# Selection passes of VectorE in another order, and weight splits ahead of GpSimd's squares, in a fused attention and expert kernel

## What is computed

```python
scores = scale * np.matmul(q, k.transpose(0, 1, 3, 2))
kth = np.partition(scores, -32, axis=-1)[..., -32:-31]
scores = np.where(scores >= kth, scores, -1e9)
attn = softmax(scores)                      # max taken off, sum + 1e-9
x = rows_of(np.matmul(attn, v))             # (2304, 512)
h = np.maximum(x @ w_in, 0.0)
x = (h * h) @ w_out                         # 512 -> 2048 -> 512
skip = x @ w_skip > 0                       # rows that go to an expert
out[skip] = x + gate * (np.maximum(x @ w1[e], 0.0) @ w2[e])
```

## Time and profile before

| | |
|---|---|
| median of 3 runs | 930.87 us (929.56 to 931.46) |
| profiled execution | 931.42 us, its span 929.7 us |
| TensorE busy | 884.4 us (95%) |
| VectorE busy | 835.4 us (90%) |
| ScalarE busy | 659.5 us (71%) |
| GpSimd busy | 656.9 us (71%) |

### The profile page before, as it was taken

How to read it: one execution, slowest core, us unless ns; L and a number is a source line. 1 busy time by engine, 2 the same in 40 slices (tenths; PEclk the granted TensorE clock), 3 DMA queues, 4 the chain that set the end, 5 groups by cost and what they waited for, 6 DMA issues and landing times.

```text
span 929.7 us, 21066 instructions
## 1 busy us (share of the span) xinstructions
PE 884.4 (95%) x6674; PEld 718.1 (77%) x6674; DVE 835.4 (90%) x2584; ACT 659.5 (71%) x1297; POOL 656.9 (71%) x884
## 2 busy tenths in 40 slices
PE   3788799999999999999999999999999999999997
PEld 1677677788788877888878887887888887688886
DVE  6999999999999999999999999999993064888887
ACT  2777777787777777778777777877876322788886
POOL 1889888777787877878788787787878443344432
PEclk9999999999999999999999999999999999999999
DMA  8962544356544567966554445633533685764990
GB/s 309 370 226 80 180 152 123 122 180 190 182 141 145 162 230 240 248 206 197 178 172 142 149 149 175 211 123 105 194 115 114 227 274 188 268 244 143 346 339 10
DMA packets 69751, 175.40 MB, mean 189 GB/s; under 512 B 21299, under 2 KB 26419, under 8 KB 65281
## 3 DMA queue, kind: packets, MB, share of 16 engines
q1 hardware_dynamic: 67792, 168.91, 54.1%
q0 software_dynamic: 1840, 5.06, 1.7%
HBM read 154.19 MB, written 21.27 MB: 189 GB/s over the span
## 4 chain that ended last, share of the span: by engine, by line
PE 59%; DVE 35%; issue 3%; POOL 1%; ACT 1%; DMA 0%; SPq 0%; POOLq 0%; DVEq 0%
DVE top L1036 11%; DVE upper L1041 10%; PE psum L1330 5%; PE psum L1395 5%; PE psum L1396 5%; PE psum L1397 5%; DVE top L1051 5%; PE psum L1412 5%; PE psum L1413 4%; PE psum L1414 4%; PE psum L1355 4%; PE psum L1374 4%; DVE lower L1056 3%; DVE lower L1027 3%; PE psum L1627 2%
## 5 line engine op out<-in xcount | busy, mean ns | idle before, releaser
L1036 DVE MAX8 top<-upper 128x8 f32<-128x288 f32 x576 | 233.3, 446 | 0.0
L620 POOL TENSOR_TENSOR s_sb<-s_sb,below 128x576 f32<-128x576 f32 x144 | 203.5, 1436 | 2.0 <-ACT below L792 2.0
L1041 DVE MATCH_REPLACE8 upper<-top,upper 128x288 f32<-128x288 f32 x432 | 187.8, 442 | 0.0
L1395 PE MATMUL psum<-x_high,w_in_high 128*128 128x256 f32 x576 | 168.4, 292 | 1.6 <-POOL x_low L626 1.1
L783 ACT ACTIVATE s_sb<-psum 128x576 f32<-128x576 f32 x144 | 93.8, 651 | 103.9 <-PE psum L1330 92.5
L1396 PE MATMUL psum<-x_low,w_in_high 128*128 128x256 f32 x576 | 161.8, 281 | 0.0
L1397 PE MATMUL psum<-x_high,w_in_low 128*128 128x256 f32 x576 | 161.2, 280 | 0.0
L635 POOL TENSOR_TENSOR square<-relu 128x256 f32<-128x256 f32 x144 | 89.8, 624 | 80.9 <-ACT relu L825 80.7
L1330 PE MATMUL psum<-k_sb,q_sb 64*128 64x288 f32 x512 | 101.3, 472 | 32.9 <-DVE lower L1027 24.0
L640 POOL TENSOR_TENSOR g_low<-square,g_high 128x256 fp32r<-128x256 f32 x144 | 108.6, 754 | 29.4 <-POOL square L635 20.4
L792 ACT ACTIVATE below<-s_sb,steep_kth 128x576 f32<-128x576 f32 x144 | 110.9, 770 | 8.3 <-POOL neg_max L608 6.7
(11 more groups left out here) (213 smaller groups left out, 1876.6 us busy)
## 6 DMA issues: line engine op xcount, KB each, us to landing
w_ring<-w_split SPq DMA_DIRECT2D x144, 512.0 KB, 4.6
weights<-w SPq DMA_DIRECT2D x32, 1024.0 KB, 6.0
v_sb<-v_main SPq DMA_DIRECT2D x48, 256.0 KB, 2.6
w_split<-w_ring SPq DMA_DIRECT2D x16, 512.0 KB, 3.1
k_sb<-kT SPq DMA_DIRECT2D x32, 144.0 KB, 4.6
k_sb<-kT SPq DMA_DIRECT2D x32, 128.0 KB, 4.4
q_sb<-qT SPq DMA_DIRECT2D x32, 128.0 KB, 4.2
weights<-w_out SPq DMA_DIRECT2D x1, 4096.0 KB, 13.4
```

The costliest lines, as they stand in the source:

```text
L620: nc.gpsimd.tensor_tensor(s_sb[:, s % SBUFS, n, 0:S], s_sb[:, s % SBUFS, n, 0:S], below[:, n, :], ALU.subtract).then_inc(masked, 1)
L1036: v.max(top[:, s % 2, n, 8 * r:8 * r + 8], upper[:, s % 2, n, :]).then_inc(upper_step, 1)
L1041: v.match_replace(upper[:, s % 2, n, :], top[:, s % 2, n, 8 * r:8 * r + 8], upper[:, s % 2, n, :], LOWEST).then_inc(upper_step, 1)
L1395: t_.matmul(dst, wh, x_high[:, j % 2, k, :], start=k == 0, stop=False)
```

## The change

Two orders change; no instruction is added or taken away.

On VectorE the last passes of step t and the first two of step t+1 are interleaved. Before, the end of a step read `upper_max(t,3,0)`, `upper_max(t,3,1)`, `pair_ranks(t)`, `invert_sums(t-1)`, `find_kth(t)`, and the next step began with `upper_max(t+1,0,0)`, `upper_max(t+1,0,1)`. After, it reads `upper_max(t,3,0)`, `upper_max(t,3,1)`, `invert_sums(t-1)`, `upper_max(t+1,0,0)`, `pair_ranks(t)`, `upper_max(t+1,0,1)`, `find_kth(t)`. The wait for `bias_set` moves with the first pass and asks for the same bounds.

On GpSimd the weight parts of a turn come ahead of the squares of its two units. Only turns 10 to 13 have both.

```diff
--- before.py
+++ after.py
@@ -702,12 +702,12 @@
                 if 0 <= t - 1 < NS:
                     mask(t - 1, 0)
                     mask(t - 1, 1)
-                for u in slots:
-                    square_low(u)
                 for f in split_parts(t, 0):
                     split_out_low(f)
                 for f in split_parts(t, FT):
                     split_in_low(f)
+                for u in slots:
+                    square_low(u)
                 if t == NS + 3:
                     set_constants()
                 if t == ENDS[GROUPS - 2] + 5:
@@ -1080,34 +1080,38 @@
 
             find_upper(0)
             find_lower(0)
-            for t in range(NS + 1):
-                if t < NS:
-
-                    wait(dve, bias_set, 2 * (t - 1))
-                    upper_max(t, 0, 0)
-                    upper_max(t, 0, 1)
-                    upper_drop(t, 0, 0)
-                    upper_drop(t, 0, 1)
-                    for r in (1, 2):
-                        upper_max(t, r, 0)
-                        upper_max(t, r, 1)
-                        lower_max(t, r - 1, 0)
-                        lower_max(t, r - 1, 1)
-                        upper_drop(t, r, 0)
-                        upper_drop(t, r, 1)
-                        if r == 1:
-                            lower_drop(t, 0)
-                            lower_drop(t, 1)
-                    if t + 1 < NS:
-                        find_upper(t + 1)
-                        find_lower(t + 1)
-                    upper_max(t, 3, 0)
-                    upper_max(t, 3, 1)
-                    pair_ranks(t)
+            upper_max(0, 0, 0)
+            upper_max(0, 0, 1)
+            for t in range(NS):
+                upper_drop(t, 0, 0)
+                upper_drop(t, 0, 1)
+                for r in (1, 2):
+                    upper_max(t, r, 0)
+                    upper_max(t, r, 1)
+                    lower_max(t, r - 1, 0)
+                    lower_max(t, r - 1, 1)
+                    upper_drop(t, r, 0)
+                    upper_drop(t, r, 1)
+                    if r == 1:
+                        lower_drop(t, 0)
+                        lower_drop(t, 1)
+                if t + 1 < NS:
+                    find_upper(t + 1)
+                    find_lower(t + 1)
+                upper_max(t, 3, 0)
+                upper_max(t, 3, 1)
                 if t >= 1:
                     invert_sums(t - 1)
-                if t < NS:
-                    find_kth(t)
+
+                if t + 1 < NS:
+
+                    wait(dve, bias_set, 2 * t)
+                    upper_max(t + 1, 0, 0)
+                pair_ranks(t)
+                if t + 1 < NS:
+                    upper_max(t + 1, 0, 1)
+                find_kth(t)
+            invert_sums(NS - 1)
 
             chain = [0]
```

## The result

The changed kernel takes 924.41 us (median of 4 runs, 924.29 to 924.70), the kernel before 931.12 in the same comparison: a ratio of 0.9928, with a 95% interval of 0.9917 to 0.9940. The forecast was 925.6 with a range of 921.8 to 928.9. In the changed file the lines of TensorE stand four further down: 1330, 1355 and 1395 are now 1334, 1359 and 1399.

A forecast was written before the change was run, and what follows sets the result against it. VectorE was taken to set the pace to about step 19, TensorE afterwards. Gains 1.1, 2.7, 0.6 and 1.1 less 0.2 make 5.3 us, giving 925.6 against the 930.87 median; likeliest 923.8 to 927.2, wider range 921.8 to 928.9.

The forecast's parts named there:

- What bounds the kernel: VectorE sets the pace to about step 19 (180 us), then TensorE, with VectorE only 0.16 us a group behind.
- The reorder: End of each VectorE step: independent instructions between dependent pairs save 0.12 us, 9.52 to 9.40; bounds 0 and 0.15.
- The rival by which the reorder would save nothing: VectorE's step stays 9.52 us and only the split's move counts, 2.7 us: 928.2; chance 0.10.
- Steps 10 to 13: Most of the `mins` stall behind GpSimd goes, 9.64 us a step: gain 2.7 us, bounds 3.7 and 1.5.
- Closing the circle through VectorE adds 0.05 (release of `mins`): Steps 10 to 13: `mins` waits for the last `g_low`; 0.05, 0.47 and 0.09 added to 9.03 give 9.64 us a step.
- "stalls vanish" rival: Steps 10 to 13: `mins` slips between GpSimd's instructions; larger late TensorE waits too; 923.3 or down to 922; chance 0.13.
- Steps 0 to 9: Later `mins` saves about 0.37 us in step 1, 0.12 each in steps 4 to 9: 1.1 us, bounds 0.5 and 1.5.
- The lateness of `kth`: While VectorE sets the pace, `kth` ending 0.59 us later against L makes TensorE's transposes about 0.2 us late once.
- wait for exponentials: In TensorE-bound steps VectorE runs ahead and waits before the reciprocal, several us in all, harmlessly.
- The late steps: TensorE loses its waits at group ends: 53 steps are 6.6 groups x 0.16 = 1.1 us.
- the three rivals that mean faster: Stalls vanish fully (0.13), VectorE's saving passes through everywhere (0.03, 919), reorder does nothing on VectorE (0.10, 928.2).
- The slower rival: Circle GpSimd, `mins`, `kth`, GpSimd decides past 9.72 us a step; at 9.81 the time is 936; chance 0.08.

The follow-up runs named there:

- reciprocal-first kernel: Kernel before with GpSimd's new order; on VectorE only the reciprocal moved ahead of `mins`, both first passes staying behind `kth`: 929.03 us, ratio 0.9975.
- VectorE's order alone: Changed kernel with GpSimd's old order put back, squares ahead of the weight parts: 926.91 us, ratio 0.9952.
- GpSimd's order alone: Kernel before with only the weight parts moved ahead of the squares on GpSimd, VectorE as before: 929.39 us, ratio 0.9983.
- the dealing 3, 2, 2: Changed kernel with weight parts dealt 3, 2, 2, then 3 x 6, 1 x 7 over the turns, instead of 4, 3 x 8, 1 x 4: 923.50 us.

## Why the prediction was right, point by point

**What bounds the kernel.** Right in what it is worth: a saving on VectorE counted nearly in full early and by about a tenth late. The border between the two parts was not where I put it, 180 us. In the kernel before, the chain that ended last stays on VectorE up to 347.81 us, so VectorE was still the one that was waited for. With TensorE's 9.62 us a step against an actual 9.64 there was next to nothing to win by that. In the changed kernel the hand-over is earlier: VectorE at 9.33 us is faster than TensorE's 9.37 as soon as the units run, the chain leaves VectorE at 105.59, and from step 13 on the score copies follow each other at TensorE's pace.

**The reorder.** The mechanism was right, its size too small: 0.2 us a step instead of 0.12. The forecast said that `kth` "already has the reciprocal between itself and `mins`" and so nothing to gain. The reciprocal-first kernel shows that reading to be wrong: `kth` waits until `mins` ends, 0.22 to 0.23 us from its start, with or without the reciprocal between them. `mins` and the reciprocal use 0.17 us of the queue in the new order, so by my estimate about 0.05 us of a second wait was saved there, beside the 0.12 ahead of `mins`; the last 0.02 is in what follows `kth`. The rival by which the reorder would save nothing fell. It went by the sentences of the Trainium skill (VectorE: DVE Perf Modes, "The DRAIN you can't avoid") that a next operation can't issue before the pipe is empty and that a semaphore costs nothing extra. The same section adds that a next operation which is not held starts earlier, which the forecast left out, and the MAX8 passes 0.365 us apart agree with that. That semaphores cost nothing is not borne out by these traces: here what waits for the result ahead of it starts 0.48 us after a MAX8 and what doesn't 0.365.

**Steps 10 to 13.** This is the mis-sized term: 2.7 us forecast, 4.0 on VectorE's clock (41.3 to 37.3). The step that failed reads "Closing the circle through VectorE adds 0.05 (release of `mins`)": `mins` was not held at all, since it started with the last `g_low` and not behind it. The bound that I gave for this, 3.7, was passed by 0.3, which is 4 x 0.07 of the shorter step; for this part it is the "stalls vanish" rival that came true, and the 924.41 of the whole lies about midway between the forecast of 925.6 and that rival's 923.3. The forecast also missed that the split at the queue's end bound TensorE through GpSimd, 9.98 us a step, whatever `mins` did. VectorE's order alone runs into that circle; GpSimd's order alone leaves `mins` against the last `g_low`. The two gains, 4.3 and 1.9, add up to 6.2; the 0.5 that is left to 6.7 lies within the intervals of the two ratios, so a gain beyond the plain sum is not shown.

**Steps 0 to 9.** Forecast 1.1 with 0.12 a step. With 0.2 a step more came, 1.5 on VectorE's clock, and still more could have: step 1 kept 1.03 us of `mins`, where 0.37 of the 1.08 was to be saved. Dealing three parts to turn 1 removed that stretch, and only the dealing 3, 2, 2 did so without a new one in steps 2 and 3.

**The lateness of `kth`.** Forecast as 0.2 us lost once. Step 9 bears it out. The lines are `upper_max(9,3,0)` and the transposes that follow, before and after:

```profile
105.45 0.81 DVE L1036 MAX8 top<-upper 128x8 f32<-128x288 f32 x2
108.30 1.09 PE L1355 MATMUL psum<-ident,s_sb 128*128 128x128 f32 x8
...
103.90 0.81 DVE L1036 MAX8 top<-upper 128x8 f32<-128x288 f32 x2
106.99 1.29 PE L1359 MATMUL psum<-ident,s_sb 128*128 128x128 f32 x8 [0.18 <-POOL s_sb L614]
```

VectorE is ahead by 1.55 us and TensorE by 1.31, so 0.24 was lost on the way. The wait for exponentials arose where the text put it and was as harmless as it said. GpSimd's waits for `kth` were forecast to grow in the early steps; they shrank, from 0.85 to 0.64 us in step 6.

**The late steps.** Forecast 1.1, measured 1.5 in the traces from 178 us on; from step 20 on, 1.0 by the kernel with the old order there.

**The sum.** By TensorE's transposes, 1.3 us were won by 108 us (forecast 1.1 - 0.2 = 0.9), 3.4 more by 149 (2.7), 0.7 more by 178 (0.6) and 1.5 after it (1.1): 7.0 of span against 5.3. Every part came out above its forecast, so the time did not land 1.2 us from the forecast, within its likeliest range of 923.8 to 927.2, by errors of both signs; only within steps 0 to 9 did one cover a part of another. The chances of the forecast and the three rivals that mean faster add up to 0.84, not 0.83. The slower rival, a circle through GpSimd and `mins` of over 9.72 us, did not come: `mins` was not held by the last `g_low`. A circle of that kind, 10.4 us a step through `mins` and the split, had bound steps 10 to 13 of the kernel before, and the change removed it.

## What to carry to other kernels

When two engines are both full, compare their periods, not their shares, and count a saving only in the stages where the engine that you relieve has the longer one; the rest turns into waiting at the first result it needs from the other. A gap ahead of a dependent instruction is filled only if every dependent pair gets independent work between it that lasts as long as the wait; one short filler for two pairs just changes places. Where a short VectorE instruction with two SBUF inputs runs beside a busy GpSimd, its place against GpSimd's instructions can be worth more than its length (here 0.2 us, and up to 1.26 when held), and the loop that GpSimd's queue forms with the other engines should be added up on its own before such a stall is blamed for a slow step.

## What the hardware showed that I had not expected

`mins` is not held when it starts with a GpSimd instruction: in steps 10 to 13 of the changed kernel it begins between 0.09 us before and 0.03 us after the start of the last `g_low` and takes 0.17 us, and that `g_low` takes 0.73 to 0.81 us and ends 0.60 to 0.65 us after `mins` does. Where it comes later than that it waits to the end of the running instruction and ends 0.04 to 0.05 us behind it. And a reciprocal of 0.15 us between two dependent instructions did not hide the wait of the second for the first: `kth` began 0.22 us after `mins` with it and 0.23 without it.
